# Banded attention in a fused float32 kernel: scores read half of a unit's keys in place, and the preparation of queries and keys is spread over the steps

## The reference

```python
# q, k, v: (2, 8, 768, 64) float32
k_sum = k.reshape(B, H, nb, block, D).max(axis=3)      # block 32: 24 summary keys
v_sum = v.reshape(B, H, nb, block, D).mean(axis=3)
scores_l = scale * np.matmul(q, k.transpose(0, 1, 3, 2))
mask_l = np.abs(pos[:, None] - pos[None, :]) < window  # window 16
scores_s = scale * np.einsum('bhsd,bhnd->bhsn', q, k_sum) + np.log(block)
scores_all = np.concatenate([np.where(mask_l, scores_l, -1e9), scores_s], axis=-1)
a = np.exp(scores_all - np.max(scores_all, axis=-1, keepdims=True))
a = a / (np.sum(a, axis=-1, keepdims=True) + 1e-09)
x = np.matmul(a, np.concatenate([v, v_sum], axis=2))
...
u = x + (np.maximum(x^T @ w_tok1, 0) @ w_tok2)^T       # token mixer
x2 = u + np.maximum(u @ w_ch1, 0) @ w_ch2              # channel mixer
...                                                    # then a gated layer: k, v, r
```

## Time and profile before

| | |
|---|---|
| median of three runs | 492.27 us (489.89, 492.27, 492.33) |
| the profiled execution, its own time | 489.64 us |
| its span in the profile | 487.9 us |
| busy over the span: PE, DVE, ACT, POOL | 467.0, 296.9, 227.4, 150.9 us |
| attention, from the start to the first `token` | 97.5 us |

### The profile page before, as it was taken

The page is one execution under the profiler, slowest core; times in us unless marked ns, Lnnn a source line. Parts: engine busy times, 40 slices in busy tenths (PEclk is TensorE's granted clock), DMA queues, the critical chain, the costliest instruction groups (busy, mean ns, idle before and its releaser), DMA issues.

```text
span 487.9 us, 7908 instructions
## 1 busy us (share of the span) xinstructions
PE 467.0 (96%) x2896; PEld 419.9 (86%) x2896; DVE 296.9 (61%) x672; ACT 227.4 (47%) x475; POOL 150.9 (31%) x155
## 2 busy tenths in 40 slices
PE   5789898999999999999999999999999999999996
PEld 4677776788999999999999999899899889989985
DVE  5789996479666665557545875666636346354511
ACT  3999995554442333413332433355544335244411
POOL 7646774260256335653326544000000000000000
PEclk9999998999999999999999999999999999999999
DMA  9999944300121212122103315310010010001001
GB/s 210 236 228 235 205 101 70 130 12 32 45 89 43 87 50 80 60 70 86 44 14 117 113 60 173 111 63 0 1 64 1 0 43 21 0 0 64 0 0 64
DMA packets 42235, 36.92 MB, mean 76 GB/s; under 512 B 20704, under 2 KB 34528, under 8 KB 42208
## 3 DMA queue, kind: packets, MB, share of 16 engines
q1 hardware_dynamic: 42208, 36.58, 27.1%
HBM read 33.43 MB, written 3.15 MB: 75 GB/s over the span
## 4 chain that ended last, share of the span: by engine, by line
PE 84%; issue 4%; ACT 4%; DVE 4%; POOL 2%; DMA 1%; ACTq 0%; DVEq 0%; POOLq 0%
PE bank L1220 19%; PE bank L1222 19%; PE bank L1221 19%; PE bank L1353 14%; PE bank L1354 7%; PE bank L1202 2%; PE bank L1272 1%; ACT e_sb L630 1%; PE bank L1168 1%; ACT qbd L610 1%; PE bank L1250 1%; DVE s_sb L868 1%; POOL xL L541 1%; DMA kn<-in_k_dram 1%; ACT kt L618 1%
## 5 line engine op out<-in xcount | busy, mean ns | idle before, releaser
L1220 PE MATMUL bank<-ucH,w1H 128*128 128x384 f32 x168 | 56.8, 338 | 0.0
L1222 PE MATMUL bank<-ucH,w1L 128*128 128x384 f32 x168 | 56.5, 336 | 0.0
L1221 PE MATMUL bank<-ucL,w1H 128*128 128x384 f32 x168 | 56.4, 336 | 0.0
L754 ACT ACTIVATE rH<-c 128x384 fp32r<-128x384 f32 x36 | 18.9, 526 | 68.6 <-DVE c L1065 68.6
L1222 PE MATMUL bank<-xkH,WkL 128*128 128x384 f32 x128 | 43.1, 336 | 0.0
L1220 PE MATMUL bank<-xkH,WkH 128*128 128x384 f32 x128 | 43.0, 336 | 0.0
L1221 PE MATMUL bank<-xkL,WkH 128*128 128x384 f32 x128 | 42.9, 335 | 0.0
L1141 DVE SCALAR_TENSOR_TENSOR k<-bank,kr 128x384 f32<-128x384 f32 x32 | 17.8, 556 | 33.4 <-ACT kr L804 33.4
L582 POOL TENSOR_TENSOR w2L<-stg,w2H 128x512 fp32r<-128x512 f32 x24 | 37.6, 1586 | 1.0
L1222 PE MATMUL bank<-WvH,k2L 128*128 128x512 f32 x96 | 37.8, 394 | 0.0
L1221 PE MATMUL bank<-WvL,k2H 128*128 128x512 f32 x96 | 37.8, 394 | 0.0
(11 more groups left out here) (142 smaller groups left out, 1209.0 us busy)
## 6 DMA issues: line engine op xcount, KB each, us to landing
stg<-in_moe_w_ch_dram SPq DMA_DIRECT2D x24, 512.0 KB, 3.4
vw<-in_v_dram SPq DMA_DIRECT2D x16, 240.0 KB, 4.3
kn<-in_k_dram SPq DMA_DIRECT2D x8, 384.0 KB, 4.5
qn<-in_q_dram SPq DMA_DIRECT2D x8, 384.0 KB, 5.5
v<-in_v_dram SPq DMA_DIRECT2D x8, 384.0 KB, 4.1
out_dram<-o_sb SPq DMA_DIRECT2D x12, 256.0 KB, 2.0
stg<-in_moe_w_k_dram SPq DMA_DIRECT2D x4, 512.0 KB, 3.4
stg<-in_moe_w_v_dram SPq DMA_DIRECT2D x4, 512.0 KB, 4.0
```

The lines of the kernel that those rows point to most:

```text
L754: act.activation(rH[slot][:, f, half * GR:half * GR + GR], src, ACT.Relu).then_inc(rh_done, 1)
L1220: pe.matmul(dst, wH, mH, start=start, stop=False, **more)
L1221: pe.matmul(dst, wH, mL, start=False, stop=False, **more)
L1222: return pe.matmul(dst, wL, mH, start=False, stop=stop, **more)
```

## The change

1. `kw` no longer holds 120 columns of each unit but 60 (`HALF`): local keys 60 to 95 and the 24 summaries. The first 60 local keys are read in place from `kt`; both lie in one tile `keys`, so that one operand of two runs of 60 columns reaches them. `kt` exists twice, for even and odd pairs.
2. VectorE copies out the keys of both heads (four copies a pair in place of two); the copy of windows, `last_keys`, has 12 x 36 columns in place of 12 x 96, and stands, with `add_summaries`, at the end of step 2 in place of step 1; `summary_keys` goes to step 2.
3. The turning is spread: head 0 of k in step 0; head 1 of k and head 0 of q in step 1; head 1 of q in step 2. ScalarE copies queries out in steps 1 and 2 and keys no more; `sum_vs` and the copy of its result go to step 0 of the pair before.
4. The high part of x is one ScalarE instruction of 768 columns, a pair later, in step 0; GpSimd's low part follows it.
5. `row_sums` is gone: the 1e-9 comes out of a further row of `aT` and `vw` (row 120: ones by 1e-9).
6. The weights of the token mixer come first product first; the first hidden tile waits for three pieces in place of six. `high_wt` is in step 0 of pairs 2 to 7.
7. At the start GpSimd makes `ident` first, then a `mask` of 3 in place of 6 patterns, and later zeroes one `qbd` and the further rows of `vw`; VectorE fills the rest. TensorE multiplies `ident` by itself six times (`WARM`), before it turns the first keys, and turns the keys of pair 1 ahead of the first scores.
8. The pairs are written out on all engines, without a hardware loop.

```diff
+    HALF = COLS // 2
+    WARM = 6
-        mask = reg.take("mask", [P, 6, COLS])
+        mask = reg.take("mask", [P, 3, COLS])
-        kw = [reg.take(f"kw{i}", [P, NU, COLS]) for i in range(2)]
-        vw = [reg.take(f"vw{i}", [COLS, NU, 2, D + 1]) for i in range(2)]
-        kt = reg.take("kt", [P, WIN + S + WIN])
+        KEYS = WIN + S + WIN
+        keys = [reg.take(f"keys{i}", [P, KEYS + NU * HALF]) for i in range(2)]
+        kt = [t[:, 0:KEYS] for t in keys]
+        kw = [t[:, KEYS:KEYS + NU * HALF].rearrange("p (t n) -> p t n", n=HALF) for t in keys]
+        vw = [reg.take(f"vw{i}", [COLS + 1, NU, 2, D + 1]) for i in range(2)]
...
         @block.gpsimd
...
+            pool.memset(qbd[1][:, :, :], 0.0).then_inc(qbd_ready, 1)
+            def last_row(par):
+                then(pool.memset(vw[par][LOC:COLS + 1, :, :, 0:D], 0.0))
+                then(pool.memset(vw[par][LOC:COLS + 1, :, :, D:D + 1], 1e-9))
...
+            last_row(0)
             sum_values(0)
             spread_vs(0, 0)
+            last_row(1)
             sum_values(1)
...
         @block.scalar
...
-                    if prep and r == 0:
-                        turn_out_k(p + 2, 2 * p + 4)
-                    if prep and r == 1:
-                        for h in range(2):
-                            turn_out_q(p + 2, par, h, 3 * p + 3)
-                    if prep and r == NG - 1:
-                        act.wait_ge(vs_spread, p + 1)
-                        turn_out_vs(p + 2, par)
-                    if r == NG - 1:
-                        act.wait_ge(norm_done, G + 2)
-                        for half, tiles in ((0, RT), (1, 1)):
...
+                    if r == 0 and p + 1 < NP:
+                        turn_out_vs(p + 1, 1 - par)
+                    if r == 0 and p >= 1:
+                        high_x(p - 1)
+                    if prep and r >= 1:
+                        turn_out_q(p + 2, par, r - 1, (bK, bQ)[r - 1])
+            def high_x(p):
+                act.wait_ge(norm_done, NG * p + NG + 2)
+                act.activation(x_halves(xH, p), x_of(p), ACT.Copy).then_inc(xh_done, 1)
...
         @block.vector
...
-            def cut_windows(par, free):
-                windows = bass.AP(kt[:, :].tensor, 0, [[2 * WIN + S, P], [UQ, NU], [1, LOC]])
-                dve.tensor_copy(kw[par][:, :, 0:LOC], windows).then_inc(kw_ready, 1)
+            def last_keys(par):
+                src = bass.AP(keys[par][:, :].tensor, HALF, [[KEYS + NU * HALF, P], [UQ, NU], [1, LOC - HALF]])
+                dve.tensor_copy(kw[par][:, :, 0:LOC - HALF], src).then_inc(kw_ready, 1)
...
-                    row_sums(G, r, gp)
-                    if prep and r == 0:
-                        turn_out_k(p + 2, 0, 2 * p + 4)
-                    elif prep and r == 1:
-                        summary_keys(p + 2)
-                    elif r == NG - 1 and 1 <= p <= NWT:
-                        high_wt(p - 1)
-                    invert(G, r)
-                    if prep and r == 0:
-                        turn_out_k(p + 2, 1, 2 * p + 4)
-                    elif prep and r == 1:
-                        cut_windows(par, 3 * p + 3)
+                    if prep and r < 2:
+                        turn_out_k(p + 2, par, r, 3 * p + 3)
+                    elif prep:
+                        summary_keys(p + 2, par)
+                    if r == 0 and 2 <= p:
+                        high_wt(p - 2)
+                    invert(G, r, gp)
                     normalise(G, p, r, gp)
-                    if prep and r == 1:
+                    if prep and r == NG - 1:
+                        last_keys(par)
                         add_summaries(p + 2, par)
-                    if r == NG - 1:
-                        high_x(G, p)
...
         @block.tensor
...
+                    unit = bass.AP(keys[par][:, :].tensor, UQ * t,
+                                   [[KEYS + NU * HALF, P], [KEYS + HALF * t - UQ * t, 2], [1, HALF]])
-                    ins = pe.matmul(bS[gp][:, COLS * n:COLS * n + COLS], qbd[par][:, t, :], kw[par][:, t, :],
+                    ins = pe.matmul(bS[gp][:, COLS * n:COLS * n + COLS], qbd[par][:, t, :], unit,
                                     start=True, stop=True)
...
+            for n in range(WARM):
+                pe.matmul(bS[0][:, 0:P], ident[:, :], ident[:, :], start=True, stop=True)
...
-                        pe.wait_ge(wl_done, NWT)
+                        pe.wait_ge(wl_done, NWT // 2 + 1)
...
-                    if prep or par == 0:
+                    if p < NP - 1:
                         scores(p + 1, 1 - par, r, 1 - gp, GU * (G + 1) + GU)
+                    if r == 0 and p + 1 < NP:
+                        pe.wait_ge(vs_read, p + 1)
+                        sum_vs(p + 1)
                     if prep and r == 0:
-                        turn_k(p + 2, par, 8 * (p - par) + 32, 5 * (p + 2))
-                    if prep and r == 1:
-                        turn_q(p + 2, par, 8 * (p - par) + 32)
-                    if prep and r == NG - 1:
-                        sum_vs(p + 2, 5 * (p + 2) + 2)
+                        pe.wait_ge(kt_written, 4 * p + 8)
+                        turn_k(p + 2, par, 0, bK)
+                    elif prep and r == 1:
+                        pe.wait_ge(vs_read, p + 2)
+                        turn_k(p + 2, par, 1, bQ)
+                        pe.wait_ge(kt_written, 4 * p + 10)
+                        turn_q(p + 2, par, 0, bK)
+                    elif prep:
+                        pe.wait_ge(kt_written, 4 * p + 12)
+                        turn_q(p + 2, par, 1, bQ)
```

More of the change, by code:

```diff
@@ L111, in build_program @@
         nmx = reg.take("nmx", [P, NG, GU])
-        sums_eps = reg.take("sums_eps", [P, NG, GU])
         rinv = reg.take("rinv", [P, NG, GU])
@@ L130, in build_program @@
         e_sb = [reg.take(f"e_sb{i}", [P, GU, COLS]) for i in range(2)]
-        aT = [reg.take(f"aT{i}", [COLS, GU, P]) for i in range(2)]
+        aT = [reg.take(f"aT{i}", [COLS + 1, GU, P]) for i in range(2)]
         reg = Region(R0, RS)
@@ new lines, in _, with turn_out_q @@
+            dve.memset(qbd[0][:, :, :], 0.0).then_inc(one_ready, 1)
+            for i in range(2):
+                dve.memset(aT[i][LOC:COLS + 1, :, :], 1.0).then_inc(aT_ready, 1)
+            def turn_out_q(pp, par, h, bank_q):
+                dve.wait_ge(q_turned, 2 * pp + h + 1)
+                dst = qbd[par][h * D:h * D + D, :, h * D + 1:h * D + D:2]
+                src = bank_q[D:2 * D, 0:NB * P].rearrange("p (u i) -> p u i", i=UQ // 2)
+                dve.tensor_scalar(dst, src, float(D) ** -0.5, None, ALU.mult).then_inc(q_written, 1)
@@ L843, in summary_keys, with turn_out_k @@
+            def turn_out_k(pp, par, h, free, first=0):
+                dve.wait_ge(k_turned, 2 * pp + h + 1)
+                if free is not None and h == 0:
+                    dve.wait_ge(scores_done, free)
+                for j in range(first, 2):
+                    dve.tensor_copy(kt[par][h * D:h * D + D, WIN + j:WIN + S:2],
+                                    (bK, bQ)[h][j * D:j * D + D, 0:NB * P]).then_inc(kt_written, 1)
+            def summary_keys(pp, par):
                 dve.wait_ge(kt_written, 4 * pp + 4)
-                dve.tensor_reduce(ks[:, :], kt[:, WIN:WIN + S].rearrange("p (n r) -> p n r", r=SUMB),
+                dve.tensor_reduce(ks[:, :], kt[par][:, WIN:WIN + S].rearrange("p (n r) -> p n r", r=SUMB),
@@ L907, in high_wt @@
                 dve.tensor_copy(hi, halves(stg[par][:, 0:512])).then_inc(wh_done, 1)
-            for j in range(2):
-                turn_out_k(0, j, None)
-            summary_keys(0)
-            cut_windows(0, None)
+            turn_out_k(0, 0, 0, None)
+            summary_keys(0, 0)
+            last_keys(0)
             add_summaries(0, 0)
+            turn_out_q(0, 0, 1, bA[1])
+            turn_out_k(1, 1, 0, None, 1)
             maxima(0, 0, 0, None)
             maxima(1, 1, 1, None)
-            for j in range(2):
-                turn_out_k(1, j, 2)
-            summary_keys(1)
-            cut_windows(1, None)
+            maxima(2, 2, 0, None)
+            summary_keys(1, 1)
+            last_keys(1)
             add_summaries(1, 1)
-            maxima(2, 2, 0, None)
             def low_h1(n):
@@ L1274, in pair @@
                     ins.then_inc(av_done, 1)
-            with pe.Fori(0, NP // 2 - 1) as i:
-                for par in range(2):
-                    pair(2 * i + par, par, True)
-            for par in range(2):
-                pair(NP - 2 + par, par, False)
+            for p in range(NP):
+                pair(p, p % 2, p < NP - 2)
             pe.wait_ge(wl_done, NWT + 1)
```

226 lines of the change are left out of this document (107 added, 119 removed).

## The result

| | before | after |
|---|---|---|
| median of four runs beside each other | 491.67 us (489.89 to 492.33) | 498.06 us (497.71 to 499.5) |
| ratio | | 1.0141, interval 1.0106 to 1.0177 |
| span of the profiled execution | 487.9 us | 496.0 us |

The change makes the kernel 1.4% slower. The forecast was 488.3 us, with a range up to 495.0.

A forecast was written before the change was run, and what follows sets the result against it. ScalarE was taken to set the pace of a pair (9.21 of 9.46 us). Terms 0.7 - 3.05 + 0.5 - 0.8 = -2.65 us gave 487.0 from 489.64, 488.3 us with half the distance to the median added; range 482.5 to 495.0.

The forecast's parts named there:

- the filled step: First filled step, pair 7's first scores to next transposes: no wait for weights, about 3.5 us for 6.55, -3.05 us.
- ScalarE idle within the pair: Sign that the forecast is right: ScalarE idle by about 1 us in each pair.
- the wait before each first scores: TensorE stands 1.65 us in every pair for VectorE's copy of summaries, 4.56 us after the start of step 2's transposes.
- The hand-over's +0.5: After pair 7: high part of x on ScalarE puts GpSimd's low part 0.55 later; +0.5 us, at least 0.
- the wait for VectorE that was to grow: At the hand-over, a token step that had already waited 0.45 us for VectorE was to wait longer.
- The failed step of the pairs: Pair loop through copies, scores and TensorE's list closes at 9.62 us, against 9.49 before; +0.7 us over five pairs.
- comes out near 8 us, not the bound: VectorE's work in a pair, after losing and gaining copies, is near 8 us and does not set the pace.
- GpSimd held up a copy: Rival: GpSimd blocks last_keys, up to 1.48 us in each loop, +7.4, in all +4.7: 495.7 us. Chance 0.07.
- The clock fell in one: Rival: clock falls at the new wait in pairs 1 to 6, 1.7 us each, +7.6: 498.5 us. Chance 0.12.
- The failed step of the start: Start: GpSimd's second sum of values ready at 18.1, pair 2's first scores at 26.8 against 27.80, -0.8 us.

The follow-up runs named there:

- runs 3: Kernel before with part 6 of the change alone (weights' order, wait for three pieces): 488.4 us, ratio 0.994.
- 12: Kernel before with part 6 of the change alone, measured again on another occasion: 487.96 us, ratio 0.9946.
- run 6: Changed kernel plus six products of ident on TensorE ahead of the first scores of pairs 2 to 7: 497.12 us, ratio 1.0142.
- Run 5: Changed kernel plus an unread reduction of 0.86 us on VectorE in step 0 of pairs 0 to 5: 503.58 us, ratio 1.0271.
- runs 1: Changed kernel with summaries, last_keys and add_summaries ahead of the maxima in step 2, not behind the division: 492.09 us, ratio 1.0014.
- 9: Kernel before with only cut_windows and add_summaries moved from step 1 to the end of step 2: 506.58 us, ratio 1.0287.
- run 7: Changed kernel, pair 0's filling behind last_keys, pair 1's behind the second tree sum, values loaded before pair 1's queries and keys: 497.88 us, ratio 1.0157.
- Runs 2: Changed kernel where GpSimd fills the further row of vw for pair 0 only after last_keys of pair 0: 500.42 us, ratio 1.0181.
- run 11: Changed kernel with keys ahead of the maxima, three start edits, and last_keys and add_summaries as reductions: 487.69 us, ratio 0.9926.
- run 10: Changed kernel with the copies last_keys and add_summaries written as reductions over an axis of one element: 495.85 us, ratio 1.0117.

## Why the prediction was wrong

- **Right**: the filled step (-2.9 for -3.05; alone, in runs 3 and 12, about 3 us of time with intervals below 1), ScalarE idle within the pair (7.81 busy of 10.02), and the wait before each first scores: 1.48 to 2.03 us for a forecast 1.65, and 4.59 to 5.15 from step 2's transposes to the scores for 4.56. The hand-over's +0.5 came out too, 0.36 of it along the chain that was named: GpSimd's low part of x began 1.71 us after the first `token` (105.03 to 106.74) in place of 1.35. But the wait for VectorE that was to grow stayed (0.44 for 0.45); a new one of 0.26, for ScalarE's turned-out tile, stands one product earlier (113.82). The rest, some 0.2, is not located.
- **The failed step of the pairs** is the sum "4.56 + 5.06 = **9.62 us**". The loop was the right one and closes at 9.94 (run 6, pair without `high_wt`). The 0.32 are almost all in TensorE's way from the first scores to step 2's transposes, 5.35 for 5.06: the four first scores, behind their wait, took 1.08 to the next start (75.67 to 76.75), where the 0.89 of the earlier trace rows had no wait ahead, and the turning 0.48 for 0.39. So 5 x (9.94 - 9.49) = 2.3 us are this loop, where +0.7 was forecast: 1.6 of the 4.5 us by which the term missed, its largest part.
- **A second step failed with it**: VectorE "comes out near 8 us, not the bound". Its busy time was 8.37, but with the copies at its end nothing covers the reply, and list plus reply are 10.02, 0.08 over the other loop. In three of the five pairs this shows, 0.2 us in all. It takes the 0.28 us by which GpSimd holds up `high_wt`: without them, by an estimate from these rows, the list would close at 9.74, under 9.94. Run 5 shows that VectorE's list takes over when it grows; runs 1 and 9 show that the place of the copies makes and unmakes the wait, in either loop.
- **Two rivals came true in part**, beside the forecast. GpSimd held up a copy in three pairs of five, and they took 0.52, 0.18 and 0.47 longer: 1.2. The clock fell in one, 1.5 (the prediction's price was 1.7). With the two steps above, 2.3 + 0.2 + 1.2 + 1.5 = 5.2. The prediction priced them as events that exclude each other and left both out of its sum; each was small, and they add.
- **The failed step of the start** is "I take the second sum as ready at 18.1, about as before". It did not follow the loads: the values' load had been moved behind the second pair's, and the first tree sum came 2.8 later, 2.45 of it waiting for that load. And the filling between the two sums, with its small one, took another 1.9 (17.75 to 19.61). Used at 22.35 in place of 18.1, the second sum is 4.25 of the 6.1 us by which the term missed. The rest is the granted clock of 0.50 over 20 to 26 us: at 1.00 the same way took 8.86 in place of 10.73 (run 7). Runs 2 and 7 show how little one link is worth there: mended alone, the first gave nothing at pair 2, and three together 2.3 us.
- **What the rest of the change is worth.** With order, start and copies mended (run 11) it can't be told from its part 6 alone in the old kernel (run 12). That the spread turning, the halved copy and the missing sum of eps gain something is not shown. The traces have pairs of 8.9 us for 9.5 (four in run 1), but no run says which part makes them; it is given back in single pairs where a blocked `high_wt` or a fallen clock costs 1 to 1.5 us.

## What to carry to other kernels

When an edit moves the producer of a value to the end of an engine's list, and the same engine next needs the consumer's answer, close every loop that passes through it: that engine's whole list and the reply behind it, whatever its busy share is, and the consumer's list. Two of them can lie 0.08 us apart, as here, and an instance that lacks one item of the list (the pair without `high_wt`) tells them apart. Take each link from a row in the same position, behind a wait if it will stand behind one. Then look whether one other item can be put behind the producer to cover the reply (three calls, 6 us here). Where DMA issues change order, follow each to the first instruction that waits for it, and expect the next link of a start to be late by nearly as much. And a rival that costs a few tenths of a microsecond in some of the periods belongs in the sum, not beside it.

## What was not expected of the hardware

- A filling by GpSimd (`MEMSET`, 25 partitions, 1.37 us) holds up a VectorE copy as its copies do: 1.63 us in place of 0.37, ending 0.25 behind it. The reverse can happen too: at 42.38 GpSimd's sum took 0.94 in place of 0.72, beside copies of 0.38 and 0.83.
- The clock did not fall at equal waits alike. After waits of 1.48 to 2.03 us it fell once in six in the changed kernel's pairs 2 to 7; with six waits of 1.83 to 1.91 (run 10, the same pairs) never; behind 2.09 us it fell in run 7 and not in run 2; behind 2.43 us (run 9) the clock was low in each of four pairs; and once it fell behind 0.95 and 0.60 us (run 11). A price per event times the number of events is a poor forecast here.
- Scores behind a wait, even a short one, took longer at the same granted clock, 1.00: the four at 75.67, behind 2.03 us of idling, 1.08 us to the next start, and as long behind 0.22 us in run 6 (73.84 to 74.92); those at 81.50, behind none, 0.89. Why is not shown.
